# A late join of each group moved from VectorE into GpSimd's next chain, with staging and masks in another order

## The reference

```python
# attention: B=4, H=8, S=768, D=48
mag = sqrt(a_re*a_re + a_im*a_im); scale = minimum(mag, 0.999) / (mag + 1e-6)
a = (a_re + 1j*a_im) * scale
for t in range(S):
    State = a[t][:, None] * State + k[t][:, None] * v[t][None, :]   # complex; k, v real
    y[t] = q[t] @ State.real
# x = y as 3072 x 384
h = maximum(maximum(x @ w1, x @ w2), x @ w3)      # 384 -> 768
x2 = h @ w_out                                    # 768 -> 384
# x2 through a router over 8 experts (top 1), each relu(x2 @ w1[e]) @ w2[e], times its gate
```

## Time and profile before

| what | value |
|---|---|
| median of 3 runs | 905.5 us (903.46 to 908.45) |
| the profiled execution | 905.75 us, span 904.0 us |
| mean granted TensorE clock | 0.96 |
| PE, PEld busy | 798.3 us (88%), 743.7 us (82%) |
| DVE, ACT, POOL busy | 640.8 us (71%), 497.1 us (55%), 481.5 us (53%) |

### The profile page before, as it was taken

One profiled execution on the slowest core, in us unless ns is written; L12 is line 12 of the kernel. 1 busy time (PEld: TensorE's weight loads), 2 busy tenths in 40 slices (PEclk: granted clock), 3 DMA queues, 4 the chain that ended last, 5 costly groups with the idle time before them and its releaser, 6 DMA issues.

```text
span 904.0 us, 18723 instructions
## 1 busy us (share of the span) xinstructions
PE 798.3 (88%) x6641; PEld 743.7 (82%) x6642; DVE 640.8 (71%) x1046; ACT 497.1 (55%) x1033; POOL 481.5 (53%) x768
## 2 busy tenths in 40 slices
PE   0659898789889999899999999949999999999995
PEld 0437787779789888888999999938999999997894
DVE  5979889799888989898887755277332353548821
ACT  5586866777767768787746564234211242437611
POOL 1197999799968797977878000002323333234222
PEclk9778999999989999999999999967999999999998
DMA  9401152452424242423322110444511142417211
GB/s 313 123 1 52 34 145 78 116 144 84 117 75 111 76 111 88 117 65 88 90 56 70 42 42 30 151 152 182 192 35 51 48 150 84 154 60 271 95 36 45
DMA packets 41875, 89.73 MB, mean 99 GB/s; under 512 B 6264, under 2 KB 23680, under 8 KB 40480
## 3 DMA queue, kind: packets, MB, share of 16 engines
q1 hardware_dynamic: 37632, 76.04, 27.5%
q0 software_dynamic: 4160, 12.60, 4.3%
HBM read 69.74 MB, written 17.69 MB: 97 GB/s over the span
## 4 chain that ended last, share of the span: by engine, by line
PE 49%; POOL 18%; DVE 14%; ACT 9%; issue 6%; DMA 2%; ACTq 0%; DVEq 0%; SPq 0%; POOLq 0%
POOL c_re L2154 6%; POOL ring L2160 4%; PE yu L1784 4%; PE yu L1788 4%; PE yu L1785 4%; POOL c_im L2158 4%; PE mm L1784 3%; PE mm L1785 3%; PE mm L1788 3%; PE tr L2056 2%; PE mm L2056 2%; PE mm L2058 2%; PE tr L2058 2%; PE tr L2057 2%; PE mm L2057 2%
## 5 line engine op out<-in xcount | busy, mean ns | idle before, releaser
L1784 PE MATMUL mm<-up_hi,x_hi 128*128 128x384 f32 x432 | 155.4, 360 | 4.9 <-ACT h_sb L792 2.7
L2154 POOL TENSOR_TENSOR c_re<-ring 112x128 f32<-112x128 f32 x165 | 121.3, 735 | 58.7 <-DVE ring L1192 42.7
L1785 PE MATMUL mm<-up_lo,x_hi 128*128 128x384 f32 x432 | 146.8, 340 | 0.0
L2239 POOL DMA_INDIRECT out_rows<-g_o,rows_out x30 | 35.2, 1174 | 145.8 <-DVE g_o L1636 137.1
L1788 PE MATMUL mm<-up_hi,x_lo 128*128 128x384 f32 x432 | 99.7, 339 | 3.4 <-DVE x_lo L1227 3.4
L2158 POOL TENSOR_TENSOR c_im<-turn,ring 112x128 f32<-112x128 f32 x105 | 77.9, 742 | 31.9 <-ACT turn L735 31.9
L1784 PEld LDWEIGHTS mm<-up_hi,x_hi 128*128 128x128 f32 x432 | 81.8, 189 | 11.3 <-issue 4.2
L2215 POOL DMA_INDIRECT g_in<-x_scratch,rows_in x34 | 37.4, 1100 | 91.2 <-DVE rows_in L1599 65.8
L1788 PEld LDWEIGHTS mm<-up_hi,x_lo 128*128 128x128 f32 x432 | 78.4, 191 | 5.0 <-DVE x_lo L1227 5.0
L1784 PE MATMUL yu<-e_hi,gh_hi 128*128 128x384 f32 x240 | 82.1, 342 | 0.0
L1785 PEld LDWEIGHTS mm<-up_lo,x_hi 128*128 128x128 f32 x432 | 81.9, 190 | 0.0
(11 more groups left out here) (264 smaller groups left out, 2347.9 us busy)
## 6 DMA issues: line engine op xcount, KB each, us to landing
...
```

The costliest lines, as they stand in the source:

```text
L1784: nc.tensor.matmul(out, hi[:, x, :], w_hi(x), start=(x == 0), stop=False)
L1785: nc.tensor.matmul(out, hi[:, x, :], w_lo(x), start=False, stop=False)
L2154: nc.gpsimd.tensor_tensor(c_re[:, 0:count, :, :], cur, bc(prev[:, :, 0, :], 2, 2), ALU.mult).then_inc(chain_prod, 1)
```

## The change

Of the three joins of a group, the last, (g, 2), is made by GpSimd for groups 4 to 11: between step 7 and step 8 of the chain of group g+1, and for group 11 behind its own chain. VectorE loses the four instructions of that join in chunk 7 and in the even chunks 8 to 20. With it go moves in the order: on ScalarE `stage_z` stands ahead of `moe_h_hi` (in chunk 7 behind it), `z_square` ahead of the rotation, the quarters 1 and 3 of the turned copies right behind `z_square` and ahead of `stage_z`, and one norm's square earlier at the start; on VectorE `mask` stands ahead of the low part of h and of the norm's end from chunk 9 on, that low part ahead of a second norm's end in chunk 2, and `z_norm` ahead of the rotation in chunks 2 and 4; the end of chunks 21 to 23 has the maxima first.

```diff
@@ tables of the joins
-        joins_head = {7: [(4, 2)], 8: [(5, 0)]}
+        joins_head = {8: [(5, 0)]}
         for g in range(5, NG):
             if g > 5:
                 joins_late[2 * g - 3] = [(g, 0)]
             joins_early[2 * g - 2] = [(g, 1)]
-            joins_late[2 * g - 2] = [(g, 2)]
+        POOLED = 4
...
-            return n in joins_late
+            return n in joins_late or 8 <= n < NC
@@ ScalarE
+            norm_square(4, norm_of(4))
             router_cols(0)
...
+                if now and n % 2 == 1:
+                    turn_quarter((n + 3) // 2, 3)
+                if more and not late_z and n != 7:
+                    stage_z(n + 1)
                 if prev2:
                     moe_h_hi(n - 2, 1)
+                if n == 7:
+                    stage_z(8)
                 for m in norms_in(n - 1) if maxima_first(n - 1) else ():
                     norm_rest(m, norm_of(m))
                 if n == 1:
                     norm_square(7, norm_of(7))
+                if n == 0:
+                    norm_rest(4, norm_of(4))
+                if more and not late_z:
+                    z_square(n + 1)
                 if now and n in (2, 4):
                     rotation(n)
-                if more and not late_z:
-                    stage_z(n + 1)
-                if n == 0:
-                    norm_rest(4, norm_of(4))
-                if now and n in (2, 4):
-                    kp_copy(n)
-                if more and not late_z:
-                    z_square(n + 1)
-                if now and (n == 0 or n >= 6):
+                if now and n % 2 == 0:
+                    turn_quarter(n // 2 + 2, 1)
+                if now and not late_z:
                     kp_copy(n)
...
-                if now and n % 2 == 0:
-                    turn_quarter(n // 2 + 2, 1)
-                if now and n % 2 == 1:
-                    turn_quarter((n + 3) // 2, 3)
@@ VectorE
+                for g, number in joins_head.get(n, ()):
+                    join(g, number)
+                if n in joins_head:
+                    moe_h_lo(n - 2, 1)
                 if maxima_first(n - 1):
                     for m in ending:
                         norm_inverse(m, norm_of(m))
-                    moe_h_lo(n - 2, 1)
-                for g, number in joins_head.get(n, ()):
-                    join(g, number)
-                for m in ending:
+                    if 8 < n < NC:
+                        mask(n)
+                    if n not in joins_head:
+                        moe_h_lo(n - 2, 1)
+                for m in ending[:1]:
+                    norm_apply(m, norm_of(m))
+                if n == 2:
+                    moe_h_lo(0, 1)
+                for m in ending[1:]:
                     norm_apply(m, norm_of(m))
...
+                if more and n in (2, 4):
+                    z_norm(n + 1)
                 if now and n >= 1:
                     rotation(n)
-                if more and n >= 2 and not late_z:
+                if more and n >= 6:
                     z_norm(n + 1)
@@ GpSimd
+            def last_join(g):
+
+                done = joins_before(g) + NBLK - 2
+                pool.wait_ge(span_step, 2 * done)
+                cur, whole = joins_of(g)[NBLK - 2]
+                re, im = (bc(bc(whole[:, y, :], 1, 2), 1, BLK) for y in range(2))
+                nc.gpsimd.tensor_tensor(l_re[0:R, :, :, :], cur, re, ALU.mult).then_inc(span_prod, 1)
+                nc.gpsimd.tensor_tensor(l_im[0:R, :, :, :], cur, im, ALU.mult).then_inc(span_prod, 1)
+                pool.wait_ge(span_prod, 2 * (done + 1))
+                nc.gpsimd.tensor_tensor(cur[:, :, 0, :], l_re[0:R, :, 0, :], l_im[0:R, :, 1, :], ALU.subtract).then_inc(span_step, 1)
+                nc.gpsimd.tensor_tensor(cur[:, :, 1, :], l_re[0:R, :, 1, :], l_im[0:R, :, 0, :], ALU.add).then_inc(span_step, 1)
...
-                chain_steps(g, range(1, most))
+                if g > POOLED:
+                    chain_steps(g, range(1, 2 * QUARTER))
+                    last_join(g - 1)
+                    chain_steps(g, range(2 * QUARTER, most))
+                else:
+                    chain_steps(g, range(1, most))
                 turns(g - 1)
                 chain_steps(g, range(most, BLK))
+            last_join(NG - 1)
             turns(NG - 1)
```

5 lines of the change are left out of this document (2 added, 3 removed).

## The result

The changed kernel takes 917.35 us (median, 915.78 to 919.78), the kernel before 905.59 us in the same session (903.46 to 908.45): ratio 1.013, 95% interval 1.0094 to 1.0166. It is slower by 1.3%, and outside the range of the prediction (893.5 to 910). The profiled execution spans 915.9 us, with a mean granted clock of TensorE of 0.952.

The account below looks back on a forecast made before the run. GpSimd, working without a pause, was to bound a pair of chunks at 41.2 us against 42.2. Terms: -3.3 to chain 9's end, -1.9 for kp stalls, +0.6 for a join: -4.6 from 905.5, so 901 us; range 893.5 to 910.

Parts of the forecast that it names:

- The join on GpSimd: GpSimd's chain: the join's four operations cost 4.1 us undisturbed plus 1.2 us of disturbance, 5.3 us; bounds 4.1 and 9.6.
- the line through the small sizes: GpSimd's operations: 2.03 ns an element on 0.20 us, giving 1.24 us for 512 elements and 0.72 for 256.
- cross-check by a ratio: GpSimd's join: at 1.96 times VectorE's time, about 2 x 2 = 4 us, agreeing with the line through the trace's sizes.
- GpSimd's pause vanishes: Steady stretch: turned quarters come sooner, so GpSimd's 5.04 us wait vanishes, leaving 37.1 us a group before the join's cost.
- The term "nothing" for the ring's load: Norm's store and ring's load (SP): the shift of 1.2 us costs nothing; 1.2 us a pair if the cover were gone.
- z and h_hi in time: Odd chunks: h_hi ready at chain end + 25.4 us, wanted at 24.8 to 25.8; just fits, costs nothing.
- TensorE's stalls: TensorE in chunks 16 and 17: stalls for kp (1.17 and some 0.75 us) go, -1.9; wait for x_lo at 1 to 2.
- Before the steady stretch: Up to chain 6: chain 5's end moves by +1.8 us, chain 6's by -0.3; chunk 7's longer wait is hidden.
- GpSimd's chain paces a pair at 41.2 us: Steady stretch: GpSimd works without a pause and sets 41.2 us a pair against 42.2; chance 0.40, for 896 to 905.
- 35.6, with what longer GpSimd operations hold it back (below), lie under this: VectorE's time a pair, 38.2 - 2.65 = 35.6 us plus holds, stays below GpSimd's 41.2 us.
- The third rival: Where q_t and k_t are made: GpSimd's long operations hold VectorE 3.1 us a pair; pair stays 42, time 905; chance 0.22.
- the 2.65 taken away: VectorE loses the join's four instructions, 683 + 858 + 520 + 591 ns = 2.65 us a pair.

Follow-up runs that it names:

- x7: The changed kernel plus 12 products of 128x384 on TensorE ahead of its wait for q_t and k_t in odd chunks 9 to 19; 912.28 us.
- x2: The kernel before with only the third late join moved to GpSimd, between step 7 and 8 of its next chain, old order kept; 921.15 us.
- x3: The changed kernel with GpSimd's join after step 9 instead of 7, and even chunks' staging of z behind h_hi; 942.97 us.
- x4: The changed kernel with each of the four operations of GpSimd's join cut into four, 16 instead of 4; 913.62 us.
- x1: The changed kernel with the join that went to GpSimd back on VectorE, new order kept (x1_join_back in full); 898.73 us.
- x12: The changed kernel with a group's middle join on GpSimd, after step 4 of the chain, and the last join back on VectorE; 899.09 us.
- after: The changed kernel itself, with the last join on GpSimd and the new order, against the kernel before; 917.35 us.

## Why the prediction was wrong

**The join on GpSimd.** Right in the mean: 5.29 us for 5.3. That it fits so well is in part luck. From first issue to last end the joins of chains 5 to 11 take from 4.02 to 6.04 us, and the third operation takes 1.36 us where 0.72 + 0.30 were summed. In chain 5 its least disturbed operations take 1.27 and 0.73 us; the line through the small sizes gave 1.24 and 0.72. (The prediction's cross-check by a ratio took 2 us for VectorE's own join, where the earlier trace rows have 2.65, so it supports the 4 us less well than it says.) GpSimd's chain operations take (762 + 664 + 627)/3 = 684 ns; over the same stretch of the kernel before it is 731 (751 in the shorter one of the earlier trace rows). That VectorE's idle time in the odd chunks is the reason is likely, not tested.

**GpSimd's pause vanishes.** Right in the main for the quarter: 31.9 us in seven chains became 12.2, though one wait of 4.0 is left. The term "nothing" for the ring's load was wrong in the changed kernel: 9.2 us of waits. In x7 they are 0.75 and 0.47. Late chunks alone do not bring them: x2, x3 and x4, whose chunks are late too, have none. Their cause stays open.

**z and h_hi in time.** Right in the steady stretch: staging waits 0.18 us for the join in chunk 13 and no more in the other odd chunks. In chunk 7 it waits 3.42 us (2.74 before), 0.7 longer where "some 2 longer" was foreseen, and I had put it down as hidden. TensorE waits 3.67 us for kp behind it in chunk 7 (3.51 in the kernel before, nothing in x1), and that chunk takes 27.7 us against 23.2 in x1, which accounts for 4.5 of the 5.6 us by which the changed kernel is behind x1 at chunk 10.

**TensorE's stalls.** Right that those for kp and x_lo go in the steady stretch.

**Before the steady stretch.** Chain 5 was to end 1.8 us later than in the kernel before and chain 6 0.3 us sooner. They ended 1.6 and 2.4 us sooner (246.0 and 288.5), and yet TensorE began chunk 10 at the same time as before, 288.6 against 288.5. So already here the end of GpSimd's chain is not what the time hangs on.

**The step that failed** is that GpSimd's chain paces a pair at 41.2 us, and in it the sentence on VectorE: "35.6, with what longer GpSimd operations hold it back (below), lie under this". A pair of chunks took 178.8/4 = 44.7 us instead, and VectorE did not wait for a chain's end in any of these chunks. The sentence sets a mean over a pair of chunks against the pace of a pair. VectorE gave up 2.65 us behind k_t, where it then stood idle 5 us and more, and was held 2.8 us ahead of k_t (6.20 against 3.39 for the decays; 1.8 in chunk 12), where it was full and the next scores wait. That it is full there could not be read from the kernel before, where it is busy 19.65 of 22.03 us in the even chunk; it follows from the change's own new order (21.36 of 21.60 in x1), for which the prediction had no term. The third rival had both the size, 3.1 us a pair, and the place, "where q_t and k_t are made, on which the next scores wait"; even piece by piece it was close (1.04 us for a product, measured 1.03 and 0.83; 0.52 for a sum, measured 0.54 and 0.41). It was lost in the next step: it set the 3.1 against the 2.65 taken away and came out at no change. Time spared in one stretch doesn't pay for time lost in another; in x12, where they are in the same one, they about cancel.

**A term that was missing** is the clock. A stall of 2.43 us was priced nowhere at more than itself, though the kernel before has stretches at 0.92 in the earlier trace rows. By x7 it costs another 6.9 us in eight chunks, and 5.1 by the medians.

**The sum, after the fact.** The medians of x1_join_back and after lie 18.6 us apart, the two profiled executions 20.6. In these, 5.6 us lie before chunk 10 and 13.0 in chunks 10 to 17. Of the 13.0, 6.9 go to the lower clock and 6.1 to the hold: even chunks lose 9, odd ones win 3 at TensorE's pace. The other 2.0 come behind chunk 17. That the first three parts make 18.6, as the medians do, is chance. The order's own gain is 4.9 us (x1 against the kernel before beside it). Both together make +13.7, where the two medians of the result are 11.8 apart; the rest is the median of the kernel before, 903.6 in one session and 905.6 in the other.

**Open.** Why x2's join costs as much as after's by another path is seen in its waits, but was not tried apart. Nor was it tried whether the clock would recover if the odd chunk's scores came in two parts. A gain of 1% came out on the way: x10_z_back, the new order without the join and with z behind h_hi, at 896.99 us, ratio 0.9899 (0.9852 to 0.9945).
